# Second layer of a three-stage kernel: seven products for eight in five of six token blocks

## What is computed

```python
def _attn_ref(q, k, v, alpha):
...
        state = alpha[:, :, t, :, None] * state + np.einsum('bhd,bhe->bhde', k[:, :, t], v[:, :, t])
        y[:, :, t] = np.einsum('bhd,bhde->bhe', q[:, :, t], state)
...
def _moe_ref(x, w_in, w_out):       # x 3072 x 384, w_in 384 x 2048, w_out 2048 x 384
    h = x @ w_in
    g = h * (1.0 / (1.0 + np.exp(-1.702 * h)))
    return (g @ w_out).astype(np.float32)
...
def _moe2_ref(x, w_in, w_out):      # the same sizes
    h = x @ w_in
    g = h - np.tanh(h)
    return (g @ w_out).astype(np.float32)
```

## Time and profile before

| | |
|---|---|
| median of 3 runs | 978.44 us (977.95 to 981.07) |
| the profiled execution: time, span of the profile | 978.98 us, 977.2 us |
| PE busy | 952.2 us (97% of the span), 9342 matmuls |
| DVE, ACT, POOL busy | 544.2, 334.1, 282.5 us |
| second layer, first tanh to last | 581.3 to 968.9 us |

### The profile page before, as it was taken

The page is one execution under the profiler, slowest core; times in us unless marked ns, Lnnn a source line. Parts: engine busy times, 40 slices in busy tenths (PEclk is TensorE's granted clock), DMA queues, the critical chain, the costliest instruction groups (busy, mean ns, idle before and its releaser), DMA issues.

```text
span 977.2 us, 22232 instructions
## 1 busy us (share of the span) xinstructions
PE 952.2 (97%) x9342; PEld 823.7 (84%) x9342; DVE 544.2 (56%) x1349; ACT 334.1 (34%) x683; POOL 282.5 (29%) x314
## 2 busy tenths in 40 slices
PE   4799999999999999999999999999999999999998
PEld 3799999999999988888888888888888888888886
DVE  7679998878888877776321224334334333343333
ACT  2342333332332332323234554333333333333332
POOL 2554656555665655444001542000000000000000
PEclk9699999999999999999999999999999999999999
DMA  7833242332332432321113322020020010200000
GB/s 159 251 76 73 57 101 55 88 76 55 95 75 55 111 65 56 102 46 23 15 62 122 98 81 89 1 65 1 1 66 1 5 60 1 65 1 1 33 1 33
DMA packets 136533, 59.07 MB, mean 60 GB/s; under 512 B 114288, under 2 KB 131824, under 8 KB 136432
## 3 DMA queue, kind: packets, MB, share of 16 engines
q1 hardware_dynamic: 133616, 55.54, 22.6%
q10 hardware_dynamic: 2816, 2.10, 0.7%
HBM read 43.45 MB, written 14.16 MB: 59 GB/s over the span
## 4 chain that ended last, share of the span: by engine, by line
PE 94%; DVE 3%; DMA 1%; SPq 1%; issue 1%; ACT 0%; DVEq 0%; ACTq 0%
PE pX L741 38%; PE pZ L765 27%; PE pX L765 14%; PE pX L618 3%; PE pX L736 2%; PE pZ L700 2%; PE pZ L645 2%; PE pZ L604 2%; PE pZ L655 1%; PE pX L631 1%; PE pZ L691 1%; DVE scores L1056 1%; DMA w_raw<-w_out 1%; DVE w_lo L1062 1%; SPq L317 0%
## 5 line engine op out<-in xcount | busy, mean ns | idle before, releaser
L741 PE MATMUL pX<-x_hi,w_hi 128*128 128x512 f32 (+2 forms) x624 | 227.7, 365 | 0.7 <-ACT g L906 0.7
L741 PE MATMUL pX<-x_lo,w_hi 128*128 128x512 f32 (+2 forms) x624 | 227.3, 364 | 0.0
L741 PE MATMUL pX<-x_hi,w_lo 128*128 128x512 f32 (+2 forms) x624 | 227.3, 364 | 0.0
L1072 DVE TENSOR_TENSOR g_lo<-g,g_hi 128x512 fp32r<-128x512 f32 (+2 forms) x208 | 133.3, 641 | 155.0 <-ACT g_hi L911 154.8
L1171 DVE TENSOR_TENSOR g<-pX,sg 128x512 f32<-128x512 f32 x96 | 66.3, 691 | 177.7 <-ACT sg L908 177.7
L765 PE MATMUL pZ<-g_hi,w_hi 128*128 128x512 f32 (+2 forms) x414 | 151.0, 365 | 0.0
L765 PE MATMUL pZ<-g_lo,w_hi 128*128 128x512 f32 (+2 forms) x414 | 150.8, 364 | 0.0
L765 PE MATMUL pZ<-g_hi,w_lo 128*128 128x512 f32 (+2 forms) x414 | 150.8, 364 | 0.0
L911 ACT ACTIVATE g_hi<-g 128x512 fp32r<-128x512 f32 (+2 forms) x208 | 121.3, 583 | 78.0 <-DVE g L1171 74.5
L906 ACT ACTIVATE g<-pX 128x512 f32<-128x512 f32 (+3 forms) x144 | 65.6, 456 | 210.1 <-PE pX L741 175.9
L741 PEld LDWEIGHTS pX<-x_hi,w_hi 128*128 128x128 f32 x624 | 117.5, 188 | 17.8 <-ACT g L906 1.1
(11 more groups left out here) (95 smaller groups left out, 1136.9 us busy)
## 6 DMA issues: line engine op xcount, KB each, us to landing
v<-v_l SPq DMA_DIRECT2D x96, 48.0 KB, 2.6
x_raw<-hidden SPq DMA_DIRECT2D x6, 768.0 KB, 5.8
attn_out<-y SPq DMA_DIRECT2D x94, 48.0 KB, 1.8
out_t<-o SPq DMA_DIRECT2D x10, 384.0 KB, 3.4
alpha<-a_t SPq DMA_DIRECT2D x24, 128.0 KB, 3.0
r<-q_t SPq DMA_DIRECT2D x24, 128.0 KB, 3.0
k<-k_t SPq DMA_DIRECT2D x24, 128.0 KB, 3.0
w_raw<-w_in SPq DMA_DIRECT2D x16, 192.0 KB, 2.4
```

Source lines behind the costliest of these rows:

```text
L741: last = nc.tensor.matmul(pH(N)[:, 0:w], win(wp, f, m), XS[T % 2][xp][:, m, 0:w], start=(n == 0), stop=(n == len(terms) - 1))
L1072: nc.vector.tensor_tensor(GL[:, columns(N)], g_raw(N), GH[:, columns(N)].bitcast(F32), ALU.subtract).then_inc(gl_done, 1)
```

## The change

For the blocks T = 9 to 13 (`paired`) the `down` products of two periods N and N + 1 (N even) are made together by `down_pair(N)`. Its operands form two 2 x 2 schemes: the weights of two slices by the output blocks m = 0 and 1, and `g` of two periods by the two halves of the 512 columns. The eight block products of such a scheme are replaced by seven, of sums of blocks, each as three matmuls of 256 columns into an accumulator of its own (`PW`, seven half banks); m = 2 stays as it was, six matmuls of 512 columns for the two periods. A pair has 27 matmuls where two `down` had 18.

The operands need sums. Of `g`, four per pair: `t_raw` (DVE, 256 columns each), then `t_hi` (ACT, 1024 columns) and `t_lo` (DVE, 1024 columns). Of the weights, four per pair of slices and once for all blocks: `s_raw` (DVE, 128 columns each), `s_hi` (ACT, 512), `s_lo` (DVE, 512), made in periods 133 to 149. At a block's end the seven accumulators are added up by `copy_paired` (DVE, seven additions of 256 columns) once ACT has copied the first of them out (`p1_copied`); ACT copies m = 2. `g` has a second buffer `g1`; pairs use the two in turn. Block 14 runs as before. POOL's `w_low2` for `w_out` waits until the sums that read the raw weights are made.

```diff
+def paired(T):
+
+    return L1B <= T < L1B + L2B - 1
...
 def products_order():
 
     order, pending = [], []
     for N in range((L1B + L2B) * NF):
         order.append(("up", N))
-        late = {128: 4, 256: 3}.get(width(N // NF), 1)
-        while len(pending) >= late:
-            order.append(("down", pending.pop(0)))
-        pending.append(N)
-    return order + [("down", N) for N in pending]
+        if paired(N // NF):
+            if N % 2 or pending[0][0] == "down":
+                order += pending
+                pending = []
+            if N % 2:
+                pending.append(("pair", N - 1))
+        else:
+            late = {128: 4, 256: 3}.get(width(N // NF), 1)
+            if not pending or pending[0][0] == "down" or N % 2:
+                while len(pending) >= late:
+                    order.append(pending.pop(0))
+            pending.append(("down", N))
+    return order + pending
...
+def place(N):
+
+    if N >= L1B * NF:
+        return N // 2 % 2, slice(N % 2 * TB, (N % 2 + 1) * TB)
     w = width(N // NF)
     n = N % NF % (2 * TB // w)
-    return slice(n * w, (n + 1) * w)
+    return 0, slice(n * w, (n + 1) * w)
...
+        GL1 = sb("g1_lo", [P, 2 * TB], F32R)
+        Tlo = [sb(f"t_lo{n}", [P, 4, TB // 2], F32R) for n in U2]
+        Slo = sb("s_lo", [P, NF // 2, 4, P], F32R)
+        GH1 = sb("g1_hi", [P, 2 * TB], F32R)
+        Thi = [sb(f"t_hi{n}", [P, 4, TB // 2], F32R) for n in U2]
+        Shi = sb("s_hi", [P, NF // 2, 4, P], F32R)
+        Gs, GHs, GLs = [G, G1], [GH, GH1], [GL, GL1]
+        SUMS = sb("sums", [P, 4, TB // 2])
...
+        PW = [pX[0][:, 2, :], pX[0][:, 3, :], pZ[0][:, 0, :], pZ[0][:, 1, :], pZ[0][:, 2, :], pZ[0][:, 3, :], pX[1][:, 2, :]]
...
+                if side:
+                    pool.wait_ge(s_step, 4 * (F // 2 + 1))
...
+            def down_pair(N):
+
+                T, f = divmod(N, NF)
+                k, n = f // 2, pair_of(N)
+                pe.wait_ge(gl_done, N + 2 - L1P)
+                pe.wait_ge(tlo_done, n + 1)
+                if T == L1B:
+                    pe.wait_ge(wlo2_done[1], f + 2)
+                    pe.wait_ge(slo_done, k + 1)
+                if k == 0:
+                    pe.wait_ge(o_copied, KC * T)
+
+                def w(F, m):
+                    return [wout(part, F, m) for part in U2]
+
+                def s_of(i):
+                    return [x[:, k, i, :] for x in (Shi, Slo)]
+
+                def g(M, h):
+                    return [at(x, M)[:, h * TB // 2:(h + 1) * TB // 2] for x in (GHs, GLs)]
+
+                def t_of(i):
+                    return [x[n % 2][:, i, :] for x in (Thi, Tlo)]
+
+                sevenths = ((w(f, 0), g(N, 0)), (w(f + 1, 0), g(N + 1, 0)), (s_of(3), g(N + 1, 1)), (w(f + 1, 1), t_of(3)),
+                            (s_of(0), t_of(0)), (s_of(1), t_of(1)), (s_of(2), t_of(2)))
+                for i, (wt, x) in enumerate(sevenths):
+                    for a, b in ((0, 0), (1, 0), (0, 1)):
+                        nc.tensor.matmul(PW[i], wt[a], x[b], start=(k == 0 and i % 2 == 0 and a + b == 0),
+                                         stop=(k == NF // 2 - 1 and b == 1), skip_group_check=True)
+                for F in (f, f + 1):
+                    wt, x = w(F, 2), [at(x, N + F - f) for x in (GHs, GLs)]
+                    for a, b in ((0, 0), (1, 0), (0, 1)):
+                        last = nc.tensor.matmul(pO[2], wt[a], x[b], start=(F == 0 and a + b == 0),
+                                                stop=(F == NF - 1 and b == 1))
+                last.then_inc(o_done, 2)
...
+                elif kind == "pair":
+                    down_pair(N)
...
+                if paired(T) and f % 2:
+                    n = pair_of(N)
+                    act.wait_ge(t2_step, 4 * (n + 1))
+                    nc.scalar.activation(Thi[n % 2][:], Traw[n % 2][:], ACT.Copy).then_inc(thi_done, 1)
...
+                        if M >= L1N:
+                            nc.scalar.activation(SUMS[:, 0, :], PW[0], ACT.Copy).then_inc(p1_copied, 1)
+                        for m in range(KC) if M < L1N else (2,):
...
+                k, odd = divmod(N - (L1B - 1) * NF - 6, 2)
+                if 0 <= k < NF // 2 and not odd:
+                    act.wait_ge(s_step, 4 * (k + 1))
+                    nc.scalar.activation(Shi[:, k, :, :], Sraw[:, k, :, :], ACT.Copy).then_inc(shi_done, 1)
...
+            def w_sums(k):
+
+                f = 2 * k
+                for F in (f, f + 1):
+                    dve.wait_ge(w2_loaded[1][F % 2], 16 * (k + 1))
+                a11, a21 = (w_raw(1, f)[:, m * P:(m + 1) * P] for m in U2)
+                a12, a22 = (w_raw(1, f + 1)[:, m * P:(m + 1) * P] for m in U2)
+                out = [Sraw[:, k, i, :] for i in range(4)]
+                nc.vector.tensor_tensor(out[0], a21, a22, ALU.add).then_inc(s_step, 1)
+                nc.vector.tensor_tensor(out[2], a11, a21, ALU.subtract).then_inc(s_step, 1)
+                dve.wait_ge(s_step, 4 * k + 1)
+                nc.vector.tensor_tensor(out[1], out[0], a11, ALU.subtract).then_inc(s_step, 1)
+                dve.wait_ge(s_step, 4 * k + 3)
+                nc.vector.tensor_tensor(out[3], a12, out[1], ALU.subtract).then_inc(s_step, 1)
+
+            def w_sums_low(k):
+                dve.wait_ge(shi_done, k + 1)
+                nc.vector.tensor_tensor(Slo[:, k, :, :], Sraw[:, k, :, :], Shi[:, k, :, :].bitcast(F32), ALU.subtract
+                                        ).then_inc(slo_done, 1)
...
+            def g_sums(N):
+
+                n = pair_of(N)
+                (b11, b12), (b21, b22) = ([g_raw(M)[:, h * TB // 2:(h + 1) * TB // 2] for h in U2] for M in (N, N + 1))
+                out = [Traw[n % 2][:, i, :] for i in range(4)]
+                dve.wait_ge(g_done, N + 2)
+                nc.vector.tensor_tensor(out[0], b12, b11, ALU.subtract).then_inc(t2_step, 1)
+                nc.vector.tensor_tensor(out[2], b22, b12, ALU.subtract).then_inc(t2_step, 1)
+                dve.wait_ge(t2_step, 4 * n + 1)
+                nc.vector.tensor_tensor(out[1], b22, out[0], ALU.subtract).then_inc(t2_step, 1)
+                dve.wait_ge(t2_step, 4 * n + 3)
+                nc.vector.tensor_tensor(out[3], out[1], b21, ALU.subtract).then_inc(t2_step, 1)
+
+            def g_sums_low(N):
+                n = pair_of(N)
+                dve.wait_ge(thi_done, n + 1)
+                nc.vector.tensor_tensor(Tlo[n % 2][:], Traw[n % 2][:], Thi[n % 2][:].bitcast(F32), ALU.subtract
+                                        ).then_inc(tlo_done, 1)
...
+            def copy_paired(T):
+
+                step = 6 * (T - L1B)
+                dve.wait_ge(p1_copied, T - L1B + 1)
                 if T > L1B:
                     dve.wait_ge(out_stored, 32 * (T - L1B))
-                nc.vector.tensor_copy(by_batch(O[:, 1, :]), pO[1][:].rearrange("p (u z t) -> p u z t", z=2, t=C)
-                                      ).then_inc(o_copied, 1)
+                _, p2, p3, p4, p5, p6, p7 = PW
+                p1, u2, u3, u4 = (SUMS[:, i, :] for i in range(4))
+
+                def out(m, h):
+                    return by_batch(O[:, m, :])[:, 2 * h:2 * h + 2, :, :]
+
+                def tokens(x):
+                    return x.rearrange("p (u z t) -> p u z t", z=2, t=C)
+
+                def add(dst, in0, in1, op=ALU.add):
+                    return nc.vector.tensor_tensor(dst, in0, in1, op)
+
+                add(u2, p1, p6).then_inc(sum_step, 1)
+                add(out(0, 0), tokens(p1), tokens(p2)).then_inc(sum_step, 1)
+                dve.wait_ge(sum_step, step + 1)
+                add(u3, u2, p7).then_inc(sum_step, 1)
+                add(u4, u2, p5).then_inc(sum_step, 1)
+                dve.wait_ge(sum_step, step + 4)
+                add(out(1, 0), tokens(u3), tokens(p4), ALU.subtract).then_inc(sum_step, 1)
+                add(out(1, 1), tokens(u3), tokens(p5)).then_inc(sum_step, 1)
+                dve.wait_ge(sum_step, step + 6)
+                add(out(0, 1), tokens(u4), tokens(p3)).then_inc(o_copied, 2)
...
+                    if not paired(T):
+                        g_low(N)
+                    elif f % 2:
+                        g_sums(N - 1)
+                        g_low(N - 1)
+                        dve.wait_ge(t2_step, 4 * (pair_of(N) + 1))
+                        g_low(N)
+                        g_sums_low(N - 1)
+                    if f == 1 and T > L1B:
+                        copy_paired(T - 1)
+                k, odd = divmod(N - (L1B - 1) * NF - 5, 2)
+                if 0 <= k < NF // 2 and not odd:
+                    w_sums(k)
+                if 0 < k <= NF // 2 and not odd:
+                    w_sums_low(k - 1)
```

More of the change, by code:

```diff
@@ L156, with same_place @@
     else:
-        BEHIND[N] = up_last
-def columns(N):
+        for M in (N, N + 1) if kind == "pair" else (N,):
+            BEHIND[M] = up_last
+def place(N):
+    if N >= L1B * NF:
```

(40 more changed lines are left out.)

19 lines of the change are left out of this document (5 added, 14 removed).

## The result

The changed kernel takes 983.93 us (median of 20, 982.57 to 986.71) against 979.2 us of the kernel before in the same session: ratio 1.0053, 95% interval 1.0046 to 1.0060. By the ratio it is 5.2 us slower, by the two medians 4.7. That is inside the range given (977.0 to 986.5) and above the 980.7 us forecast.

A forecast was written before the change was run, and what follows sets the result against it. PE, busy 97% of the span, was taken to bound the kernel. A saving of 8.2 us against waits of 0.2, 1.0, 3.45 and 5.8 gave +2.2 us, so 978.44 + 2.2 = 980.7 us; range 977.0 to 986.5.

The forecast's parts named there:

- The saving: PE's matmuls in 40 pairs: 3.88 us per pair in place of 4.08, -8.2 us in all.
- The rival of a better pace: Narrow matmuls in pairs start closer than 119.8 ns, at 113.3: 976.7 us, or 972.9 with shorter DVE operations; chance 0.16.
- The chain: DVE and ACT operations from the odd period's g to the end of t_lo, 3.93 us, before PE can start a pair.
- block ends: Ends of blocks T = 10 to 13: PE waits 0.24 us for DVE's additions, four times, +1.0 us.
- the list of signs: What the later profile would show: start distances, DVE busy time, and PE's waits at opening pairs, block ends and N = 224.
- The rival of a longer chain: DVE's operations before a pair and at block ends take longer than laid out: 984.0 to 987.4 us; chance 0.16.
- the opening: Start of layer 2, pairs 144 to 150: missing cover and weight sums make PE wait, +5.8 us together.
- slice 6: In each of four blocks x_hi and x_lo go ahead of the odd period's g: 0.05 us each, +0.2 us.
- The wait into block 14: At N = 224 PE waits for ACT's copy and DVE's seven additions with no up between: +3.45 us.
- the likeliest case: Whole kernel: +2.2 us to 980.7 us, own range 977.9 to 982.4, clock staying at 1.00; chance 0.44.
- The clock rival: The granted clock falls in the wait into block 14, costing 3.4 us more: 984.0 us, slower by 0.6%; chance 0.24.
- The hidden edits: Weight sums in periods 133 to 143, POOL's wait for s_step and SP's later store: claimed to cost PE nothing.

The follow-up runs named there:

- e3: Changed kernel with the sums of weights left out, pairs reading plain weight parts instead; 982.13 us, ratio 1.0043 to the kernel before.
- e7: Changed kernel with pairs in blocks 10 to 13 only, block 14's products three periods behind, down(159) behind up(161); 973.63 us, ratio 0.9946 to before.
- e10: Changed kernel, pairs still from block 9, with block 14's products three periods behind and down(143) behind up(145); 978.46 us, ratio 0.9995 to before.
- e2: Changed kernel with block 14's products three periods behind instead of one; 978.62 us, ratio 0.9995 to the kernel before.
- e4: Changed kernel with block 9 given its plain products back, pairs in blocks 10 to 13 only; 981.40 us, ratio 1.0026 to the kernel before.
- e5: Changed kernel with each pair's six 512-column matmuls ahead of its 21 of 256 columns; 985.68 us, ratio 1.0065 to the kernel before.
- e1: Changed kernel with 14 filler matmuls of 512 columns ahead of block 14's first product; 982.26 us, ratio 1.0038 to the kernel before.
- e6: Changed kernel with the edits of e4 and e2 together; 976.15 us, ratio 0.9968 to the kernel before.
- e8: Changed kernel without pairs or sums, plain products, block 14's products three periods behind; 982.35 us, ratio 1.0035 to the kernel before.

## Why the prediction was right, and where it was off

*The saving.* 119.8 ns per narrow matmul was right to 0.2 ns, so layer 1's rows priced a stream of other operands well, and the 109.2 ns by the Trainium skill (TensorE: Matmul & The Clock Gate, Back-to-back issue gap), an estimate from its formula for the gap of an isolated matmul, was too low here. The rival of a better pace is out. What I had not priced are the wide matmuls behind a narrow burst: +1.1 us.

*The chain.* 3.93 us from `g` to the end of `t_lo` against 3.95 measured, and from it the waits: 1.9, 1.4, 0.5 and 1.6 forecast, 1.80, 1.24, 0.42 and 1.53 measured; 0.24 at block ends against 0.26. up(147), which has 0.4 in the sum but is missing from the list of signs, lost 0.30 and 0.11 at its second matmul. The rival of a longer chain is out: a DVE operation of 256 columns takes 0.42 as in the earlier trace rows in all 40 pairs, and POOL, beside whose `w_lo` DVE was slower in the earlier trace rows, cost nothing visible here: its four `w_lo` of 591.40 to 595.67 fell where DVE stood idle or read PSUM, but for the end of an `s_lo` that took its usual 0.68. (The POOL row ends just before that `g_lo` starts; three more `w_lo` follow it at once, up to 549.19, and it is beside them that the `g_lo` ran.) The causes of the opening were two, as laid out: weight sums (e3) and missing cover. That cover takes the wait away is shown at the opening of block 10 (e7); at that of block 9 the same shift brought other waits with it (e10). Per block, slice 6 came out 0.05 and block ends 0.1 higher, since a restarted pair's second matmul comes 0.20 us after the first and not 0.12; timeline of PE, kernel after:

```profile
746.06 0.39 PE L787 MATMUL pX<-x_lo,w_hi 128*128 128x512 f32 x1
746.31 0.36 PE L843 MATMUL pX<-g_hi,w_hi 128*128 128x256 f32 x1
746.51 0.28 PE L843 MATMUL pX<-g_hi,w_lo 128*128 128x256 f32 x1
```

*The wait into block 14.* 3.45 forecast, 3.48 measured, and e2 shows that it was bare, not needed.

*The step that failed* is the choice of the likeliest case. I took the clock to stay at 1.00 through that wait and gave its fall 0.24. It fell, at 3.3 us of idleness, in the profiled execution of the changed kernel and in those of e3, e4 and e5, which have the same wait, and in none of e1, e2, e6, e7 and e10, which don't stand still there, nor in e8, whose longest waits there are 1.5 us. Its price was mis-sized as well: 3.4 us from the 6.8 us stretch of the earlier trace rows, measured 1.6, since the low stretch was 3.4 us long. So with the right case and the right size the sum would have been +3.8, and with the wide matmuls +4.9.

*Luck.* The likeliest case, +2.2, missed the measured 5.46 by over 3 us, more than its own range allowed. The clock rival's +5.6 meets it, and by luck: its clock was 1.8 us too dear, and the wide matmuls (1.1) and the slower second distance behind each wait (0.7 at slice 6, block ends and block 14), for which it had no term, made that up.

The hidden edits were hidden: N = 128 to 144 takes the same 65.28 us, and SP and POOL are named in no wait of PE in the second layer.

## What to carry to other kernels

Price an exchange of matmuls by the distance of starts at each width, then list the places where the usual cover is missing: the first use, the last use, and each seam; here they cost some 12.7 us (the table's rows from slice 6 down) against 8.2 saved, and e7's three changes (no pairs in block 9, later products in block 14, down(159) later) brought 10 back. Here a copy hidden under one product became a copy and seven additions of 3.1 us together (910.94 to 914.08), which needed two; the order can put them there. And the longest wait was dearer than its length: 3.5 us of waiting, and 1.6 us of lower clock behind it.
